# Attention and two feed-forward layers on one core: the 1e-9 of the softmax sums on VectorE behind the output sum, and 34 turns of the identity ahead of head 1

## The reference, cut to what matters

```python
def _attn_ref(q, k, v, w1, b1, w2):              # q, k, v: (4, 8, 576, 64)
    scores = scale * np.matmul(q, k.transpose(0, 1, 3, 2))
...
    scores = scores + bias.transpose(2, 0, 1)[None, :, :, :]
    scores = scores - np.max(scores, axis=-1, keepdims=True)
    attn = np.exp(scores)
    attn = attn / (np.sum(attn, axis=-1, keepdims=True) + 1e-09)
    return np.matmul(attn, v).astype(np.float32)

x = attn_out.transpose(0, 2, 1, 3).reshape(B * S, H * D)     # 2304 x 512
h = x @ w_in;  r = np.maximum(h, 0.0);  x = (s * (r * r) + b) @ w_out
h = x @ w_in2; x = (h - np.tanh(h)) @ w_out2
```

## Time and profile before

| | |
|---|---|
| median of 3 runs | 1090.35 us (1090.28 to 1091.12) |
| the profiled execution | 1089.92 us |
| its span, first to last instruction | 1088.1 us |
| TensorE busy | 1050.2 us, 97% |
| ScalarE busy | 728.4 us, 67% |
| GpSimd busy | 690.6 us, 63% |
| VectorE busy | 625.1 us, 57% |

### The profile page before, as it was taken

How to read it: one execution, slowest core, us unless ns; L and a number is a source line. 1 busy time by engine, 2 the same in 40 slices (tenths; PEclk the granted TensorE clock), 3 DMA queues, 4 the chain that set the end, 5 groups by cost and what they waited for, 6 DMA issues and landing times.

```text
span 1088.1 us, 16872 instructions
## 1 busy us (share of the span) xinstructions
PE 1050.2 (97%) x5685; PEld 912.5 (84%) x5685; DVE 625.1 (57%) x1128; ACT 728.4 (67%) x1469; POOL 690.6 (63%) x656
## 2 busy tenths in 40 slices
PE   6679999999999999999999999999999999999998
PEld 2168889888888888888888888888888888999998
DVE  7968877655775475567747755761450451440640
ACT  8978888767878587777758766873562553552652
POOL 1056666687778778868876887766454455455553
PEclk9999999999999999999999999999999999999999
DMA  5788867799889788998996799764333333333331
GB/s 191 252 251 261 269 196 175 198 253 230 211 214 259 205 210 237 238 212 196 255 268 164 184 274 245 186 145 134 106 116 98 99 115 125 119 121 101 96 122 64
DMA packets 185338, 201.19 MB, mean 185 GB/s; under 512 B 125811, under 2 KB 129829, under 8 KB 185253
## 3 DMA queue, kind: packets, MB, share of 16 engines
q1 hardware_dynamic: 185108, 200.04, 67.2%
q10 hardware_dynamic: 144, 0.07, 0.1%
HBM read 155.23 MB, written 15.64 MB: 157 GB/s over the span
## 4 chain that ended last, share of the span: by engine, by line
PE 70%; ACT 14%; issue 7%; DVE 6%; DMA 2%; POOL 1%; SPq 0%; DVEq 0%; ACTq 0%; POOLq 0%
PE ps_f L919 19%; PE ps_f L921 19%; PE ps_f L920 19%; ACT x_raw L345 2%; PE ps_o L555 2%; DVE g_buf L979 2%; PE ps_s L594 2%; ACT planes L642 2%; ACT gh L932 2%; DVE g_buf L982 2%; PE ps_s L595 1%; PE ps_o L558 1%; PE ps_o L570 1%; ACT ps_t L654 1%; ACT gh L936 1%
## 5 line engine op out<-in xcount | busy, mean ns | idle before, releaser
L876 POOL TENSOR_TENSOR wl<-w_raw,wh 128x512 fp32r<-128x512 f32 x318 | 418.3, 1320 | 255.9 <-ACT wh L869 254.8
L919 PE MATMUL ps_f<-gh,wh 128*128 128x464 f32 (+1 forms) x640 | 242.7, 379 | 2.3 <-DVE g_buf L979 1.7
L919 PE MATMUL ps_f<-xh,wh 128*128 128x464 f32 (+1 forms) x640 | 240.5, 376 | 0.6 <-DVE ptl L748 0.6
L921 PE MATMUL ps_f<-xh,wl 128*128 128x464 f32 (+1 forms) x640 | 237.4, 371 | 0.0
L920 PE MATMUL ps_f<-gl,wh 128*128 128x464 f32 (+1 forms) x640 | 237.4, 371 | 0.0
L921 PE MATMUL ps_f<-gh,wl 128*128 128x464 f32 (+1 forms) x640 | 237.2, 371 | 0.0
L920 PE MATMUL ps_f<-xl,wh 128*128 128x464 f32 (+1 forms) x640 | 237.1, 370 | 0.0
L869 ACT ACTIVATE wh<-w_raw 128x512 fp32r<-128x512 f32 x318 | 196.6, 623 | 48.4 <-PE ps_f L921 48.2
L919 PEld LDWEIGHTS ps_f<-gh,wh 128*128 128x128 f32 x640 | 120.8, 189 | 16.0 <-DVE g_buf L979 2.8
L919 PEld LDWEIGHTS ps_f<-xh,wh 128*128 128x128 f32 x640 | 120.5, 188 | 13.4 <-DVE ptl L748 0.8
L921 PEld LDWEIGHTS ps_f<-xh,wl 128*128 128x128 f32 x640 | 120.1, 188 | 13.4
(11 more groups left out here) (126 smaller groups left out, 1694.8 us busy)
## 6 DMA issues: line engine op xcount, KB each, us to landing
w_raw<-in_w_out SPq DMA_DIRECT2D x80, 512.0 KB, 3.6
w_raw<-in_w_in SPq DMA_DIRECT2D x79, 512.0 KB, 3.5
bias_t<-bias_flat SPq DMA_DIRECT2D x128, 288.0 KB, 4.0
bias_flat<-stage SPq DMA_DIRECT2D x36, 295.5 KB, 2.2
k_raw<-in_kt SPq DMA_DIRECT2D x32, 288.0 KB, 4.1
q_raw<-in_qt SPq DMA_DIRECT2D x32, 288.0 KB, 3.6
v_raw<-in_vt SPq DMA_DIRECT2D x22, 288.0 KB, 3.2
bias_t<-bias_flat SPq DMA_DIRECT2D x32, 144.0 KB, 4.3
```

The source lines that it names most:

```text
L876: pool.tensor_tensor(wl[:, b % RING, :, :], raw_block(b), wh[:, b % RING, :, :].bitcast(F32), ALU.subtract).then_inc(w_lo_done, 1)
L919: pe.matmul(acc, hi, rhs_h[:, k0 + kk, 0:T], start=(first and kk == 0), stop=False)
L921: mm = pe.matmul(acc, lo, rhs_h[:, k0 + kk, 0:T], start=False, stop=(last and kk == 3))
```

## The change

The sum den + 1e-9 for the reciprocal is made by VectorE and no longer by ScalarE, and both it and the reciprocal stand behind the head's output sum (L797) on VectorE, where the reciprocal stood ahead of it. The second edit turns the identity 34 times into ps_f behind the scores of step 4, the last tile of head 0, and ahead of the scores of head 1.

```diff
@@ act_step
-            if t == 0 and turning(n):
-                v = n - 1
-                need(act, inv_done, v)
-                act.wait_ge(exp_done, (v + 1) * NT)
-                act.activation(den_e[:], den[:, v % 2, :], ACT.Copy, bias=1e-9).then_inc(den_done, 1)
@@ dve_step
-            if t == 1 and turning(n):
-                v = n - 1
-                dve.wait_ge(den_done, v + 1)
-                need(dve, inv_turned, v)
-                dve.reciprocal(inv[:], den_e[:]).then_inc(inv_done, 1)
             if j is not None and j % NT == NT - 1:
...
                                          op0=ALU.mult, op1=ALU.add).then_inc(o_done, 1)
+            if t == 1 and turning(n):
+                v = n - 1
+                dve.wait_ge(exp_done, (v + 1) * NT)
+                dve.tensor_scalar(den_e[:], den[:, v % 2, :], 1e-9, None, ALU.add).then_inc(den_done, 1)
+                dve.wait_ge(den_done, v + 1)
+                need(dve, inv_turned, v)
+                dve.reciprocal(inv[:], den_e[:]).then_inc(inv_done, 1)
@@ block.tensor
             for g in STEPS_AT[:FIRST]:
                 pe_step(pe, g, True)
+                if g == NT - 1:
+                    pe_idle_turns(pe, ps_f, 34)
```

## The result

The changed kernel takes 1091.75 us (median of 22 runs, 1090.84 to 1094.35) against 1090.53 us for the kernel before (22 runs): a ratio of 1.0014, with a 95% interval of 1.0008 to 1.0019. It is 0.14% slower: a small change, but clear of zero, and within the 0.2% that I called no change; 1090.9 us was forecast. Its profiled execution took 1091.35 us. One further execution of the kernel before, beside the first experiments, took 2074.41 us in a slow state and is left out of every ratio and count.

A forecast was written before the change was run, and what follows sets the result against it. TensorE, busy 97%, bounds the kernel; the stage before the rounds is a TensorE-VectorE ring. Median 1090.35 us, - 0.56 for the clock, + 1.08 for six heads gave about 1090.9 us, range 1089.5 to 1092.5.

The forecast's parts named there:

- The turns are hidden and cost nothing: Behind step 4's scores, 34 turns of 0.11 us (3.7 us) fit in TensorE's 4.29 us wait, ending about 66.5.
- They keep the clock: Turns count as activity, leaving TensorE idle 0.5 us instead of 4.3; granted clock 1.00 from 66 to 70 us.
- The gain of 0.56 us: Steps 5 and 6 at full clock, limited by ScalarE's wait for q: 0.56 us gained, bounds 0 and 0.89.
- ScalarE's copy comes 0.10 us earlier: Without den_e on ScalarE, copy o_tmp and the output sum come 0.10 to 0.22 us earlier a head; 0.10 taken.
- The tail on VectorE: Sum and reciprocal between output sum and next minimum: 0.28 us, net 0.18 us a head, bounds 0 and 0.40.
- Six heads pay: Of eight heads before the rounds, two swallow the delay in waits for q and inv_b; 6 x 0.18 = 1.08 us.
- + 0.52: Whole kernel: clock gain - 0.56 plus tail cost + 1.08 gives + 0.52 us, about 1090.9 us.
- the rival in which the clock falls: In the gap after step 4's scores the clock falls despite the turns: 1091.4 us, chance 0.10.

The follow-up runs named there:

- 68 turns: Changed kernel with 68 identity turns in place of 34: median 1094.57 us of 5 runs, ratio 1.0034 to the kernel before.
- turns alone: Kernel before with only the 34 identity turns added, the 1e-9 staying on ScalarE: median 1089.53 us of 12 runs, ratio 1.0000 to the kernel before.
- 40 turns: Changed kernel with 1e-9 left out of the first ten heads and 40 turns for 34: median 1090.23 us, ratio 0.9992 to the kernel before.
- move alone: Changed kernel without the turns, only sum and reciprocal moved: median 1092.45 us of 8 runs, ratio 1.0020 to the kernel before.
- the kernel without the sum: Changed kernel with 1e-9 left out of the first ten heads, reciprocal ahead of the output sum: median 1090.57 us, ratio 0.9995 to the kernel before.
- the two repeats: Changed kernel measured twice more, nothing altered, for further traces: ratios 1.0024 and 1.0018 to the kernel before.
- the tail ahead of the output sum: Changed kernel with VectorE's sum and reciprocal put back ahead of the output sum: median 1093.51 us of 11 runs, ratio 1.0030 to the kernel before.
- the sum made earlier: Changed kernel with VectorE's 1e-9 sum one step earlier, reciprocal again ahead of the output sum: median 1093.0 us, ratio 1.0017 to the kernel before.
- the four sums: Changed kernel with four more same-size sums into an unread tile, in the tail: median 1096.03 us of 6 runs, ratio 1.0046 to the kernel before.

## Why the prediction held, and where a size was off

- **The turns are hidden and cost nothing: right.** Forecast 62.7 to 66.5, seen 62.33 to 66.20. The 68 turns show the price beyond the wait.
- **They keep the clock: right in nine of ten traces.** The trace does not agree with the rule that the prediction cites from the Trainium skill, TensorE: Matmul & The Clock Gate, section "Part 4: PE-mode transpose", since nothing but turns filled the gap and the clock held. What I left out is that the gap is not the same each time: from the end of the scores of step 4 to those of step 5 it is 4.29, 4.60 and 4.27 us in the kernel before and 4.36 to 4.66 us in the eight other traces with 34 or 40 turns, but 5.20 in the turns alone, where the clock fell.
- **The gain of 0.56 us: right, as far as one trace tells.** Between the changed kernel and the one trace of the move alone A to D differs by 0.60, of which 0.2 to 0.6 us may be that trace's sum in step 6, drawn out to 0.78 us. The gain is limited by the transfer of q, as forecast, in the first pair of traces (0.91 us at step 6, 0.53 at L743). That limit was seen in the changed kernel each time (the wait for q was 1.42, 1.90 and 1.46 us), but in the kernel before only in the trace I had (0.49 us, and none in the other two).
- **ScalarE's copy comes 0.10 us earlier: right**, twice over (the head above, and the kernel without the sum).
- **The tail on VectorE: a size off by 0.04 us.** The sum is 0.15 to 0.17 us, the own semaphore 0.03 to 0.04, the reciprocal 0.19, and the minimum starts 0.07 before its end. I left out the 0.03 us between the end of the output sum and the start of the sum. From output sum to minimum it is 0.35 us, where I expected 0.28 in the profile; it was 0.03 before, so the tail adds 0.32. My sum took 0.28 for the added time too and did not take off that 0.03. A head grows by 0.22 and not by 0.18.
- **Six heads pay: this is the term that was mis-sized.** I let two heads swallow the delay in a longer wait. The one behind inv_b is there in every trace, but takes up only half, on the mean: that distance is 10.30, 9.97 and 9.97 us before and 10.20, 10.21 and 10.19 after. The one behind q (9.70 us in the trace I had) is 9.34 and 9.33 in the two other traces of the kernel before: it was chance. B to C grows from 66.51 to 67.88, by 1.38 us over seven distances, and C to D by 0.31, which holds the tail of the eighth head. That is 1.69 us. The first head's earlier copy, 0.10 us, lies in A to B, so 1.59 stands against my 1.08 and - 0.59 against my - 0.56.
- **The sum.** - 0.69 (A to B) + 1.38 + 0.31 = + 1.00 us by the traces, against + 0.52. The first measurement says + 0.9 to + 2.1 us, the two repeats + 1.0 to + 3.8: the forecast had the direction right and the size within 0.2%, but its + 0.52 lies below all three, and one of the two waits that it counted on was there by chance. The total alone would fit the rival in which the clock falls (1091.4 us) as well as the forecast; the traces decide against it. What the measurements may hold above 1.00 us goes, in the first measurement, with the executions whose clock is below 1.000, of which the changed kernel has no trace; I can't name an instruction for it.
- **A mechanism I had not forecast:** in step 6 the sum on VectorE took 0.56 us behind GpSimd's rounding of k (70.73 to 71.39). In the changed kernel one of ten sums meets this in the first trace, none in the second and two in the third (0.29 and 0.50 us); in the other heads of the first GpSimd is waiting for q or inv_b at that time.

## What to carry to other kernels

In a ring of two engines a small instruction costs its place, not its engine's load: directly ahead of the instruction that the other engine waits for it is paid in full, 0.32 us a head here (0.22 net of the 0.10 that ScalarE gave back), though VectorE is busy 57% of the span. A slack read from one trace has to be asked twice: waits for transfers came and went from trace to trace, and a delay that hides behind one is a gain by chance. Before an elementwise operation goes to VectorE, look at what GpSimd does at that time, and prefer the form of instruction that did not wait for it here.

## What the runs showed of the hardware that I had not expected

A tensor_scalar of 128x5 on VectorE waits for a GpSimd instruction that is under way, to its end: 0.67, 0.85 and 1.03 us in the tail ahead of the output sum, and 1.20 us in the sum made earlier, against 0.15 to 0.17 alone. Sixteen sums in all traces took over 0.2 us, and each ended 0.02 to 0.03 us after the end of a GpSimd instruction that was under way when it started. The reciprocal of the same size took 0.17 to 0.19 in every trace, also in the 33 cases in which GpSimd was at work as it started.

The Trainium skill says so of the tensor_scalar in SBUF — State Buffer, section "Who interferes with whom": a tensor_scalar can use the ports that VectorE shares with GpSimd, and of two instructions that want them the one that comes second is blocked until the first is done. The trace agrees, with those ends 0.02 to 0.03 us apart.

TensorE's clock can fall with work under way: at about 70.3 us in the turns alone, 1.5 us after TensorE had gone on at full clock from an idle time of 1.48 us, and at 233.06 us in the trace of the four sums, 0.7 us after an idle time of 2.30 us. An idle time of 2.02 us that ended at 227.93 in the turns alone was followed by no fall.
